# A causal convolution with two feed-forward layers: the second layer's factor moved from weights to activations, one tile split earlier, identity turns added

## The reference

```python
def _attn_ref(x, weight_gen):                  # x [2, 4096, 192], weight_gen [2, 4096, 8, 7]
    w = weight_gen - np.max(weight_gen, axis=-1, keepdims=True)
    w = np.exp(w)
    w = w / (np.sum(w, axis=-1, keepdims=True) + 1e-09)
    ...
    out = np.einsum('bshk,bskhg->bshg', w, x_unf)      # causal, 7 taps, 8 heads of 24
def _moe_ref(x, w_in, w_out):                  # w_in [192, 2048], w_out [2048, 192]
    h = np.maximum(x @ w_in, 0.0)
    return (h * h @ w_out).astype(np.float32)
def _moe2_ref(x, w_in, w_out):
    h = x @ w_in
    g = h * np.cos(h)
    return (g @ w_out).astype(np.float32)
```

## Time and profile before

| | |
|---|---|
| median of three runs | 1194.85 us (1194.55 to 1198.56) |
| the profiled execution | 1197.12 us, span 1195.3 us |
| its mean granted clock of TensorE | 0.996 |
| busy: TensorE matmul, weight load | 1174.2 us (98%), 1107.3 us (93%) |
| busy: VectorE, ScalarE, GpSimd | 964.0 us (81%), 815.5 us (68%), 365.8 us (31%) |

### The profile page before, as it was taken

One profiled execution on the slowest core, in us unless ns is written; L12 is line 12 of the kernel. 1 busy time (PEld: TensorE's weight loads), 2 busy tenths in 40 slices (PEclk: granted clock), 3 DMA queues, 4 the chain that ended last, 5 costly groups with the idle time before them and its releaser, 6 DMA issues.

```text
span 1195.3 us, 25441 instructions
## 1 busy us (share of the span) xinstructions
PE 1174.2 (98%) x9768; PEld 1107.3 (93%) x9768; DVE 964.0 (81%) x1503; ACT 815.5 (68%) x1488; POOL 365.8 (31%) x265
## 2 busy tenths in 40 slices
PE   6999999999999999999999999999999999999998
PEld 4978999899999999999999999999999999999976
DVE  7867888978878787787878878787787878878787
ACT  3987675766667676676766666666666767666675
POOL 3894706061250704206060240705216070000000
PEclk8999999999999999999999999999999999999999
DMA  7422111011111111111001111101111000100000
GB/s 191 116 67 48 35 27 34 10 19 35 28 34 18 28 23 23 34 27 35 12 17 35 27 34 22 35 13 22 34 28 34 13 16 3 26 1 15 1 15 14
DMA packets 113172, 37.30 MB, mean 31 GB/s; under 512 B 101662, under 2 KB 110878, under 8 KB 113052
## 3 DMA queue, kind: packets, MB, share of 16 engines
q1 hardware_dynamic: 111100, 34.87, 13.9%
q10 hardware_dynamic: 1952, 0.80, 0.3%
HBM read 23.84 MB, written 6.29 MB: 25 GB/s over the span
## 4 chain that ended last, share of the span: by engine, by line
PE 90%; DVE 5%; ACT 3%; issue 1%; DMA 0%; SPq 0%; ACTq 0%; DVEq 0%
PE y L593 47%; PE h L593 43%; DVE h L1345 1%; DVE h L1367 1%; DVE g_lo L1380 1%; DVE turns L1349 1%; ACT turns L1076 1%; ACT g_hi L1089 1%; ACT relu L1049 0%; ACT arena L1032 0%; DMA xc<-in_x_dram 0%; DVE x L1322 0%; ACT gen L1038 0%; DVE stat L1205 0%; DVE stat L1196 0%
## 5 line engine op out<-in xcount | busy, mean ns | idle before, releaser
L593 PE MATMUL y<-g_hi,wo 64*128 64x512 f32 x3048 | 699.4, 395 | 0.6 <-DVE y_part L1389 0.4
L593 PE MATMUL y<-g_lo,wo 64*128 64x512 f32 x2032 | 526.2, 393 | 0.0
L593 PEld LDWEIGHTS y<-g_hi,wo 64*128 64x128 f32 x3048 | 423.4, 184 | 27.2 <-PE y L593 5.1
L514 POOL TENSOR_TENSOR tap<-xc,gen 128x768 f32<-128x768 f32 x98 | 150.9, 1546 | 581.9 <-DVE xd_lo L1357 566.3
L593 PEld LDWEIGHTS y<-g_lo,wo 64*128 64x128 f32 x2032 | 309.0, 184 | 4.8
L1076 ACT ACTIVATE turns<-turns 128x512 f32<-128x512 f32 x238 | 150.4, 632 | 197.1 <-DVE turns L1349 196.2
L593 PE MATMUL h<-xa_hi,wa_hi 64*128 64x512 f32 x1016 | 273.9, 400 | 2.9 <-issue 2.4
L593 PE MATMUL h<-xa_lo,wa_hi 64*128 64x512 f32 x1016 | 269.8, 393 | 0.2 <-DVE g_lo L1239 0.2
L593 PE MATMUL h<-xa_hi,wa_lo 64*128 64x512 f32 x1016 | 268.2, 391 | 0.0
L1367 DVE TENSOR_TENSOR h<-h,turns 128x512 f32<-128x512 f32 x238 | 165.9, 697 | 122.5 <-ACT turns L1076 121.6
L1345 DVE SCALAR_TENSOR_TENSOR h<-h,relu 128x512 f32<-128x512 f32 x249 | 173.4, 697 | 66.2 <-ACT relu L1049 63.6
(11 more groups left out here) (117 smaller groups left out, 1093.8 us busy)
## 6 DMA issues: line engine op xcount, KB each, us to landing
xc<-in_x_dram SPq DMA_DIRECT2D x60, 240.0 KB
out_dram<-arena SPq DMA_DIRECT2D x62, 64.0 KB, 1.9
xt_a<-x_blocks SPq DMA_DIRECT2D x224, 16.0 KB, 1.8
arena<-in_moe_w_out_dram SPq DMA_DIRECT2D x16, 192.0 KB, 3.1
arena<-in_moe_w_in_dram SPq DMA_DIRECT2D x16, 128.0 KB, 2.4
out_dram<-arena SPq DMA_DIRECT2D x62, 32.0 KB, 1.7
xt_d<-x_blocks SPq DMA_DIRECT2D x112, 16.0 KB, 1.8
arena<-in_moe_w_in_dram SPq DMA_DIRECT2D x16, 64.0 KB, 2.9
```

What stands on the lines that cost most here:

```text
L514: pool.tensor_tensor(tap[:, k % 2, :].rearrange("p (r g) -> p r g", g=GROUP), rows[k], wk, ALU.mult).then_inc(pool_step, 1)
L593: return pe.matmul(o, w[rows, :], x[rows, :], start=start, stop=stop)
```

## The change

1. *The factor.* The second layer's weights are split as they are (L1032 goes, and `by`). 1/(2 pi) is put on the second layer's x where it is split (`x2_part`, `x2_high`, `sum_y1`, `x2_low`), 2 pi on g where it is split (ScalarE's Copy gets a scale; VectorE's subtraction becomes a `scalar_tensor_tensor` that multiplies and subtracts).
2. *Tile 1's split* is in slot 13 (was 14), and behind the slot's own high and low halves (`x1_highs`, `x1_lows`).
3. *Slot 19* makes the first layer's halves (`high`, `low`) before the second layer's first turns.
4. *Identity turns* (`keep_busy`): 8, 7, then 8 for each of four sums, 6 more behind the last of these, 2 between the two turns of tile 0's x, 3 inside slot 0. They write another bank of `h`.
5. *The last step* of the second layer is done in two halves of 256 tokens (`parts`, `last_tail_up`, `last_down` and the tail's ScalarE and VectorE code).

```diff
@@ -86,7 +87,7 @@
 
     def split_at(t):
 
-        return (SLOTS - 2, SLOTS - 5)[t] if t < PEEL else SPLIT
+        return (SLOTS - 3, SLOTS - 5)[t] if t < PEEL else SPLIT
 
     def y1_at(t):
 
...
@@ -299,6 +298,12 @@
         def downs_in_halves(n):
 
             return n + 1 - (n > CATCH_UP - D1)
+
+
+        def parts(m):
+
+            count = 2 if m == STEPS - 1 else 1
+            return [(k, slice(k * TOK // count, (k + 1) * TOK // count)) for k in range(count)]
 
         def wait_squared(eng, n):
 
...
+            def keep_busy(count):
+
+                for _ in range(count):
+                    pe.transpose(h[:, 3, 0:P], ident[:, :], ident[:, :])
...
@@ -618,6 +628,7 @@
                     pe.wait_ge(piece_ready[0], 1)
                 pe.matmul(o, wa_lo[l][:, f_cols], xa_hi[l][:, par, :], start=False, stop=False)
                 if first:
+                    keep_busy(3)
                     pe.wait_ge(x1_split, 1)
                 pe.matmul(o, wa_hi[l][:, f_cols], xa_lo[l][:, par, :], start=False, stop=False)
                 if first:
...
+            def last_tail_up(m, k):
+
+
+                f, of = m % SLOTS, m // SLOTS % 2
+                (o, cols), (o2, cols2) = [(h[:, tail_bank(m + part), :], at) for part, at in parts(m)]
+                down = (y1, 1, k % SLOTS, g2_hi[:, k % 2, :], g2_lo[:, k % 2, :])
+                turn = k - (TAIL - LAG - TAIL_D2) + 1
+                up_a(o, 1, f, of, BOTTOM, 0, cols, start=True)
+                up_a(o, 1, f, of, BOTTOM, 1, cols)
+                end_of_tail_up(m - 1)
+                up_a(o, 1, f, of, BOTTOM, 2, cols)
+                up_d(o, 1, f, of, 0, cols)
+                pe.wait_ge(g2_ready, k + 1)
+                pe.wait_ge(tail_a_done, turn - 1)
+                down_a(down, TOP, 0)
+                up_d(o, 1, f, of, 2, cols).then_inc(h2_left, 1)
...
+                pe.wait_ge(h2_left, m)
+                up_a(o, 1, f, of, TOP, 0, cols)
+                up_a(o, 1, f, of, TOP, 1, cols)
+                pe.wait_ge(tail_a_left, turn)
+                down_a(down, BOTTOM, 0)
+                up_a(o, 1, f, of, TOP, 2, cols)
+                up_d_top(o, f, cols, stop=True).then_inc(up2_done, 1)
+                down_a(down, BOTTOM, 1)
+                down_d(down, TOP, 1).then_inc(tail_d_left, 1)
+                down_a(down, BOTTOM, 2).then_inc(tail_a_done, 1)
+                pe.wait_ge(h2_left, m + 1)
+                up_a(o2, 1, f, of, TOP, 0, cols2)
+                up_a(o2, 1, f, of, TOP, 1, cols2)
+                pe.wait_ge(tail_d_left, turn)
+                down_d(down, BOTTOM, 0)
+                up_a(o2, 1, f, of, TOP, 2, cols2)
+                up_d_top(o2, f, cols2, stop=True).then_inc(up2_done, 1)
+                down_d(down, BOTTOM, 1).then_inc(down2_done, 1)
...
@@ -997,14 +1063,17 @@
                         turn_x1(1, part)
 
             pe.wait_ge(ident_ready, 2)
-            pe.wait_ge(first_product, 1)
-            for k in range(TAPS - 2):
-                if k:
-                    pe.wait_ge(first_sum, k)
-                for _ in range(WARM_UP):
-                    pe.transpose(h[:, 0, 0:P], ident[:, :], ident[:, :])
+
+            for k in range(2):
+                pe.wait_ge(first_product, k + 1)
+                keep_busy(8 - k)
+            for k in range(1, TAPS - 2):
+                pe.wait_ge(first_sum, k)
+                keep_busy(8)
+            keep_busy(6)
             pe.wait_ge(first_sum, TAPS - 1)
             turn_x1(0, 0)
+            keep_busy(2)
             pe.wait_ge(first_sum, TAPS + 1)
             pe.wait_ge(pad_zeroed, 1)
             turn_x1(0, 1)
@@ -1024,13 +1093,9 @@
                 cols = slice(q * PIECE, (q + 1) * PIECE)
                 rows = slice(l * DD, (l + 1) * DD)
                 act.wait_ge(piece_loaded[r], 48 * (pc // RING + 1))
-                by = (2.0 * math.pi if op == 2 else INV_2PI) if l else 1.0
                 hi, w = [(wa_hi[l][:, cols], stage_a[:, r, :]), (wd_hi[rows, cols], stage_d[rows, r, :]),
                          (wo[l][:, q * PF:(q + 1) * PF, 0:DM], stage_o[:, r, :, :])][op]
-                last = act.activation(hi, w, ACT.Copy, scale=by)
-                if l:
-                    last = act.activation(w, w, ACT.Copy, scale=by)
-                last.then_inc(piece_hi[pc], 1)
+                act.activation(hi, w, ACT.Copy).then_inc(piece_hi[pc], 1)
 
             def exps(part):
 
@@ -1050,20 +1115,17 @@
                     if n in ACT_SQUARES:
                         act.wait_ge(relu_done, n + 1)
                         act.activation(h1_bank(n), relu[:, b, :], ACT.Square).then_inc(early_square, 1)
+                if m == 0:
+                    high(n)
                 if live(m):
                     act.wait_ge(up2_done, m + 1)
                     if counted(m - 1):
                         act.wait_ge(g2_made, m - 1)
                     act.activation(turns[:, c, :], h2[c], ACT.Copy,
                                    bias=0.25).then_inc(turns_ready, 1)
-                if i == split_at(t) and tile_live(t + 1):
-                    if t == 0:
-                        act.wait_ge(x1_turned, 4)
-                    else:
-                        act.wait_ge(blocks_moved, MOVE * t)
-                    for part in range(2):
-                        act.activation(by_half(x1_high(1 - par, part)), x1_source(t + 1, part),
-                                       ACT.Copy).then_inc(x1_hi_ready, 1)
+                if i == split_at(t) and t > 0 and tile_live(t + 1):
+                    act.wait_ge(blocks_moved, MOVE * t)
+                    x1_highs(t, par)
                 if i == y1_at(t) and t > 1:
                     x2_part(t, par)
                 if i == Y2_AT and tile_live(t - 2):
-                if live(n):
-                    act.wait_ge(relu_done, n + 1)
-                    if before_in_bank(n) >= 0:
-                        act.wait_ge(down1_done, before_in_bank(n) + 1)
-                    act.activation(g1_buffers(n)[0], relu[:, b, :], ACT.Square).then_inc(g1_hi_ready, 1)
+                if live(n) and m != 0:
+                    high(n)
+                if i == split_at(t) and t == 0:
+                    act.wait_ge(x1_turned, 4)
+                    x1_highs(t, par)
                 if live(m):
                     act.wait_ge(g2_made, m + 1)
                     if counted(m - D2 + 1):
                         act.wait_ge(down2_done, m - D2 + 1)
-                    act.activation(g2_hi[:, c, :], h2[c], ACT.Copy).then_inc(g2_hi_ready, 1)
+                    act.activation(g2_hi[:, c, :], h2[c], ACT.Copy, scale=2.0 * math.pi).then_inc(g2_hi_ready, 1)
...
+            def high(n):
+
+                act.wait_ge(relu_done, n + 1)
+                if before_in_bank(n) >= 0:
+                    act.wait_ge(down1_done, before_in_bank(n) + 1)
+                act.activation(g1_buffers(n)[0], relu[:, n % 2, :], ACT.Square).then_inc(g1_hi_ready, 1)
+
+            def x1_highs(t, par):
+
+                for part in range(2):
+                    act.activation(by_half(x1_high(1 - par, part)), x1_source(t + 1, part),
+                                   ACT.Copy).then_inc(x1_hi_ready, 1)
+
             def x2_part(t, par):
 
                 act.wait_ge(y1_d_done, SLOTS * t)
                 if counted(t - 1):
                     act.wait_ge(x2_split, t - 1)
-                act.activation(y1_part, first_sums(t - 1)[0:DD, 1, :], ACT.Copy).then_inc(y1_part_ready, 1)
+                act.activation(y1_part, first_sums(t - 1)[0:DD, 1, :], ACT.Copy,
+                               scale=INV_2PI).then_inc(y1_part_ready, 1)
...
-                act.activation(xa_hi[1][:, 1 - par, :], first_sums(t - 1)[:, 0, :], ACT.Copy).then_inc(x2_hi_ready, 1)
+                act.activation(xa_hi[1][:, 1 - par, :], first_sums(t - 1)[:, 0, :], ACT.Copy,
+                               scale=INV_2PI).then_inc(x2_hi_ready, 1)
...
@@ -1344,6 +1428,8 @@
                     dve.wait_ge(relu_done, n + 1)
                     dve.scalar_tensor_tensor(h1_bank(n), h1_bank(n), 0.0, relu[:, b, :], ALU.max,
                                              ALU.mult).then_inc(square_ready, 1)
+                if m == 0:
+                    low(n)
                 if live(m):
                     dve.wait_ge(turns_ready, m + 1)
                     dve.scalar_tensor_tensor(wave[:, c, :], h2[c], 0.25, turns[:, c, :], ALU.add,
-                if live(n):
-                    wait_squared(dve, n)
-                    dve.wait_ge(g1_hi_ready, n + 1)
-                    hi, lo = g1_buffers(n)
-                    dve.tensor_tensor(lo, h1_bank(n), hi, ALU.subtract).then_inc(g1_ready, 1)
+                if live(n) and m != 0:
+                    low(n)
+                if i == split_at(t) and t == 0:
+                    x1_lows(t, par)
                 if live(m):
                     dve.wait_ge(g2_hi_ready, m + 1)
```

(4 more changed lines are left out.)

126 lines of the change are left out of this document (80 added, 46 removed).

## The result

| | before | changed |
|---|---|---|
| median | 1195.8 us (6 runs, 1194.29 to 1198.56) | 1189.54 us (6 runs, 1189.38 to 1189.70) |
| the profiled execution | 1197.12 us, span 1195.3 | 1189.38 us, span 1187.6 |

The ratio is 0.9944, 95% interval 0.9929 to 0.9959: 0.6% faster. Forecast were 1188.7 us, and 1189.4 for the profiled execution.

What follows compares the result with a forecast made beforehand. TensorE was taken to set the pace in the long middle. Terms 3.1 + 1.6 + 0.6 + 0 + (2.8 - 0.4) + 0 = 7.7 us took 1197.12 to 1189.4, and 0.7 carried over gave 1188.7; range 1186.4 to 1192.0.

Steps and rivals of the forecast that it cites:

- The clock: Slots 1 and 2: extra identity turns hold the clock at full, saving 3.1 us (bounds 0 and 3.4).
- The copies: Slots 21 to 27: removing 24 ScalarE copies brings them to TensorE's pace, saving 2.79 us; 0.57 more at slots 17 and 18.
- The 0.57 at slots 17 and 18: Slots 17 and 18: 0.57 us counted as lost beyond the products' time, to go with the ScalarE copies.
- The split: Slot 16: its 1.62 us wait for tile 1's last low half goes whole when the split moves to slot 13.
- Slot 19's order: Slots 19 and 20: first-layer halves first; slot 20's 1.26 us loss stays, gain 0 (bounds 0 and 0.3).
- VectorE's new wait: Third tile's x transpose: VectorE waits 0.4 to 0.5 us for GpSimd's sum; 0.4 charged (bounds 0 and 4.8).
- The last step: End of kernel: halves shorten the chain about 0.9 us, extra products cost as much; gain 0 (bounds 1.0 gained, 0.5 lost).
- From the profiled execution to the median: Whole kernel: of the profiled execution's 2.3 us above the median 1194.85, 0.7 is carried over, 1189.4 to 1188.7.
- the clock falls anyway: Rival, kernel start: the clock drops despite the turns, 3.1 us is missing, 1190.2 up to 1192.5; chance 0.20.
- half-width products are cheap: Rival, last step: half-width products cost little, or the whole 2.3 offset carries over, 1187 us; chance 0.12.
- VectorE waits longer for the convolution: Rival, third tile: GpSimd's sum ends near 90, VectorE waits 2.5 us; 1190.5, at most 1193; chance 0.17.
- The subtraction with a factor: Slower rival, middle slots: VectorE's 238 subtractions could be slow for rounded output, at 1.6 us giving 1209; chance 0.02.

Runs made afterwards that it cites:

- the square: Four kernels with the new turns and whole last step: with copies 1194.41 us (split in slot 14), 1194.71 (slot 13); without copies 1191.72, 1190.46.
- the levels: 71 runs of the unchanged kernel before: 29 at 1194.1 to 1194.8 us, 12 near 1196.8, 20 from 1197.7 to 1198.6, 10 near 1199.9.

## Why the prediction came out right, and where its steps did not

The span is the 1187.6 that the sum gave, but some terms cancelled. In the trace it is 2.99 (clock) + 0.41 (x's load, luck) - 0.59 (slot 6) + 1.64 (split) + 0.11 + 2.53 (copies) + 0.54 (behind slot 28) = 7.63 up to the transpose, where the sum had 7.7.

- *The clock*: 3.1 forecast, 2.99 measured in the profiled execution, 2.40 after slot 6. It holds for such an execution alone; on the fastest of before the turns gain nothing. The cover that I named ("both idled while slots 1 and 2 crawled") was wrong: 0.59 came back at slot 6. The reading "at its full level (2.4 GHz) up to about 22.4 us" was wrong for the first turns (1.94 us for eight against 1.09).
- *The copies*: 2.79 forecast for slots 21 to 27, 2.53 measured, 31.34 against the 31.08 of full pace. The 0.57 at slots 17 and 18 was no loss: with the copies gone slot 18's matmul still follows slot 17's by 4.30. I had priced the five full-height products by their own spacing (0.23 to 0.31, 65.41 to 66.42 in the changed kernel) and left out what passing into and out of full height costs: 0.54 us from the last half-height product to the first full-height one, and 0.32 back. The 0.54 is 0.53 to 0.55 in nine profiles, whether VectorE's last low half is done 0.05 or 0.5 us ahead of the weight load, so it is no wait for VectorE. With it, the spacing's 2.19 us of loss between 60 and 80 was too much, and TensorE's idle time of 1.53, which I had set aside, lay nearer to the 1.64 gained.
- *The split*: 1.62 forecast, 1.64 at slot 16. With the copies it is worth nothing; it needed their removal, and I had named that only as a help. Its price and the copies' were given as if they could be added, and the square says that they can't.
- *Slot 19's order*: 0 forecast, 0.13 the other way, within the runs' spread.
- *VectorE's new wait*: 0.4 charged, none measured. The sum ended at 88.26 (forecast 87.7), and VectorE came at 88.58 (87.3): VectorE gained 5.9 us up to there, where I had 7.2.
- *The last step*: 0 taken of 1.0 to be had; 0.85 to 0.92 by the medians, 0.61 to 0.68 by the end of the traces. A mis-sized term, near its upper bound.
- *From the profiled execution to the median*: of the 2.3 by which the profiled execution stood above the median I carried over 0.7, from 1189.4 to 1188.7. The changed kernel's profiled execution lies at its median, and so the forecast is 0.8 too low. The guess behind it, that the distance is the clock's, is what the levels show; the right use was that a kernel which holds the clock has no such levels, so nothing is carried over. The median of before moves with the draw: 1194.85 from three runs, 1195.8 from six. Against its fastest level, 1194.4, the change gains 4.9 us.

Of the rivals, that the clock falls anyway is out for these turns, but for one execution: of 63 of the changed kernel and its variants with all of them, 62 have a mean clock of 0.999 or 1.000 and their usual time, and one ran at half pace (last section). With five turns fewer it is what happens. My argument against it, that the clock had stayed up across 0.27 and 1.05 us, was weak: the fall at 22.4 stands behind the 1.05 and behind gaps of 0.40 and 0.46 that I didn't name, and the variant without five turns reopens just such small ones. The rival that half-width products are cheap came true for its part, the last step. That VectorE waits longer for the convolution came true only when 0.3 us more was gained ahead of it. The subtraction with a factor takes 690 ns, the plain one 679, both rounded outputs:

```profile
L1462 DVE SCALAR_TENSOR_TENSOR g_lo<-h,g_hi 128x512 fp32r<-128x512 f32 x238 | 164.1, 690 | 16.6 <-ACT g_hi L1151 0.8
L1473 DVE TENSOR_TENSOR g_lo<-h,g_hi 128x512 fp32r<-128x512 f32 x256 | 173.8, 679 | 1.8 <-issue 0.5
```

## What to carry to other kernels

Waits on different engines in neighbouring slots cover one another: before adding up two gains, ask whether the stall that one removes is where the engine of the other catches up, and test the corners, not only each change alone. A kernel whose runs fall on distinct levels may lose its clock at the start in some executions; fill the gaps up to and inside the first real product too, and judge by many runs, since one profile can't show it. Each step forward moves into the next wait, which here was 0.3 us away (GpSimd's sum) or behind a buffer that had to come free sooner.
